# The eighth expert's vector loaded by DMA for every chunk, and the first chunk's state products in two groups

## Chip, cores and metric

One core of one Trainium2 chip (trn2) runs the whole kernel. The metric is device microseconds (us) of one execution; the median of three executions is compared. The profile is one further execution.

## What is computed

Three layers in a row. A linear attention with a decaying state (4 batches, 8 heads, 768 positions, head size 64), a two-layer network (512 to 2048 to 512) with a learned slope for negative values, and a mixture of 8 experts in which each of the 3072 tokens goes to the expert whose embedding has the largest cosine with it:

```python
state = gamma[None, :, None, None] * state + np.einsum('bhd,bhe->bhde', k[:, :, t], v[:, :, t])
y[:, :, t] = scale * np.einsum('bhd,bhde->bhe', q[:, :, t], state)
...
g = np.maximum(h, 0.0) + alpha * np.minimum(h, 0.0)
...
en = expert_emb / (np.linalg.norm(expert_emb, axis=-1, keepdims=True) + 1e-06)
logits = xn @ en.T / tau
expert_idx = np.argmax(logits, axis=1)
...
h = np.maximum(x[mask] @ w1[e], 0.0)
out[mask] = gate_w[mask, None] * (h @ w2[e])
```

## The kernel before

**Stages.** The 768 positions are cut into six chunks (c = 0 to 5) of 128 positions by 4 batches, 512 tokens each. For each chunk TensorE does the attention (`attention`, heads in four pairs, hp = 0 to 3) and then the network (`mlp`, 16 blocks, f = 0 to 15). In a block TensorE does `hidden(c, f + 1)`, 12 matmuls at L750, and then `down(c, f)`, 12 matmuls at L768. Every product is taken of a high and a low part of the numbers, so VectorE, ScalarE and GpSimd make such parts all the time. After chunk 5 come the experts (L843 to L903), some 350 us.

**A block outside TensorE.** VectorE forms `neg` (L1034) and `g` (L1039) from the result of `hidden`, ScalarE copies the high part `g_hi` (L1533, semaphore gh), GpSimd subtracts for the low part `g_lo` (L1784, semaphore gl; VectorE does it in blocks 0 and 15). `down(c, f)` waits for gh before its first matmul and for gl before its fifth.

**The first chunk** (no state yet) also splits the network's weights, one slab n per block: SP loads slab n (`load_w`, L479) into one of two buffers, ScalarE takes the high part (`split_w`, L1509) in block n - 3 behind `g_hi`, VectorE the low part (L985) in the same block. `load_w(n)` waits until slab n - 2 is split. Between blocks TensorE inserts `to_state(0, hp)` (L678), which makes keys times values into the state product of a pair of heads, in a PSUM bank (6 or 7); semaphore SU counts them. VectorE copies each to the state `St` one block later (L1054, semaphore S).

**SP's queue** is one list of transfers in written order, each with its waits ahead of it, so one that waits holds all behind it. In the first chunk `load_w` for n = 4 to 15 is mixed with the next keys and values:

```python
                if n in (7, 10, 13, 15):
                    u = 2 + (7, 10, 13, 15).index(n)
                    load_k(u // HP, u % HP)
                if n in (7, 10, 13):
                    load_v(1, (7, 10, 13).index(n))
```

`load_k` for u = 2, 3, 4, 5 waits for SU of 1, 2, 3, 4 state products, since these read the buffer that it fills. The `load_v` after n = 7, 10, 13 waits for the same count as the `load_k` ahead of it.

**The router** of chunk c runs in the network of chunk c + 1. VectorE takes the dot product of each token with each expert's normalized vector: 32 instructions `scalar_tensor_tensor` of 128x512 (`dots`, L1098), two in blocks 0 and 8, four in blocks 1 to 7. The vectors of experts 0 to 6 lie in SBUF, the same in all 128 partitions, in `EN`. They are written to DRAM by the first chunk (`en_rows`) and loaded with a broadcast once (`spread_en`, L522), in chunk 1. That of expert 7 lies in PSUM (`EN_ps`, bank 7), put there by one matmul (L817) between the first chunk's network and `attention(1)`. The dots write their product, which nobody reads, to `dot_out`, the two halves of the mask buffer `Am`; the sum goes to `L2`. Squares of the rows are taken by ScalarE.

Of the kernel before, what the change touches and what calls it, by code (L numbers as in the profile page):

```python
# [23 lines left out]
P = 128  # L24
# [49 lines left out]
def build(nc, g, where, qk, kv, w_mlp, alpha, emb, tau, w_exp, consts, pad_rows, en_rows, table, out):  # L74
# [10 lines left out]
    TB = B * P  # L85
# [93 lines left out]
    St = part(HP * B * D).rearrange("p (h b c) -> p h b c", h=HP, b=B)  # L179
    assert at[0] == 13 * TB  # L180
    idle_in = A[:, 11 * TB:11 * TB + P]
    dot_out = [A[:, (9 + i) * TB:(10 + i) * TB] for i in range(2)]
    EN = sb("en_all", (E - 1) * DM, f32)
    v_first = by_batch(EN[:, 0:TB])
    qk_first = [EN[:, (1 + 2 * i) * TB:(3 + 2 * i) * TB] for i in range(2)]
# [113 lines left out]
    RK_last = bank[3][:, 0:B * E].rearrange("p (b e) -> p b e", b=B)  # L299
    CNT_first, CNT_ps = bank[6][:, 64:64 + E], bank[7][:, 64:64 + E]  # L300
    SQ_ps = bank[6][:, :]
    EN_ps = bank[7][:, :]
    EMB_ps = bank[5][:, 192:192 + KC * E].rearrange("p (k e) -> p k e", k=KC)
    TAU_ps = bank[5][:, 256:257]
    XT_ps, EH_ps, HT_ps, EY_ps = bank[6], [bank[4], bank[5]], [bank[0], bank[1]], [bank[2], bank[3]]
# [119 lines left out]
    LO_VECTOR_AT = {11: 0, 12: 1, 13: 2, 14: 3}  # L425
    STAR_AT, TURN_AT = 13, FB - 2

    SU_AT = {1 + 3 * hp: hp for hp in range(HP)}

    block = nc.Block()  # L430
    with block:

        @block.sync
        def _(sp):
# [77 lines left out]
                if n in (7, 10, 13):  # L512
                    load_v(1, (7, 10, 13).index(n))
            sp.wait_ge(s_en, due(s_en, 1))
            sp.dma_start(en_rows[0:E - 1, :], emb_sb[0:E - 1, :]).then_inc(s_en_st, 16)
            sp.wait_ge(s_en_st, due(s_en_st, 16))
            sp.wait_ge(s_SU, due(s_SU, HP))
            sp.wait_ge(s_Y, due(s_Y, HP))
            sp.wait_ge(s_en_last, due(s_en_last, 1))

            def spread_en():
                sp.dma_start(EN[:, :], en_rows[0:E - 1, :].rearrange("e d -> (e d)").partition_broadcast(P))\  # L522
                  .then_inc(s_en_all, 16)
                sp.dma_start(table[PAD:PAD + P, :], pad_rows[0:P, :]).then_inc(s_pad0, 16)

            def chunk(c, following=True, with_k=True):

                load_qk(c, 2)
                load_qk(c, 3)
                load_v(c, 3)  # L530
                if following:
                    load_k(c, 2)
                    load_k(c, 3)
                    load_qk(c + 1, 0)
                    load_v(c + 1, 1)
                    load_qk(c + 1, 1)
                if isinstance(c, int) and c == 1:
                    spread_en()
                if following:
                    if with_k:  # L540
                        load_k(c + 1, 0)
                    load_v(c + 1, 2)
                    if with_k:
                        load_k(c + 1, 1)
                    load_v(c + 1, 0)

            chunk(1)
            for e in range(E):
# [76 lines left out]
        def _(pe):  # L625
# [148 lines left out]
            def mlp(c, router_c=None):  # L774


                hidden(c, 0)
                for f in range(FB):
                    if f + 1 < FB:
                        hidden(c, f + 1)  # L780
                    if f == 0 and not is_last(c) and not (isinstance(c, int) and c == 0):
                        pe.wait_ge(s_S, due(s_S, HP * c + HP))
                    down(c, f)
                    if isinstance(c, int) and c == 0 and f in SU_AT:
                        if SU_AT[f] >= 2:
                            pe.wait_ge(s_S, due(s_S, SU_AT[f] - 1))
                        to_state(0, SU_AT[f], SU0_ps[SU_AT[f] % 2])
                    if f == RANK_AT and router_c is not None:
                        router_rank(router_c)

                    if f == RANK_AT + 4 and router_c is not None:
                        pe.wait_ge(s_rk, due(s_rk, router_c + 1))
                    if is_last(c) and f == TURN_AT:
                        pe.wait_ge(s_lg, due(s_lg, B * E * (NC - 1)))
                        x_transpose(0, 0)
                        x_transpose(0, 1)
# [17 lines left out]
            for kc in range(KC):  # L814
                tr(EMB_ps[:, kc, :], emb_sb[0:E, kc * P:(kc + 1) * P], ident[0:E, 0:E])
            mm(TAU_ps, ones[0:1, :], tau_in[0:1, :], start=True, stop=True).then_inc(s_emb, 1)
            mm(EN_ps, ident[0:E, E - 1:E].broadcast_to([E, P]), emb_sb[0:E, :], start=True, stop=True).then_inc(s_en_last, 1)  # L817
            pe.wait_ge(s_ent, due(s_ent, 1))
            pe.wait_ge(s_S, due(s_S, HP))
            attention(1)  # L820
# [128 lines left out]
            e = e_next  # L949
# [27 lines left out]
        def _(dve):  # L977
# [50 lines left out]
            def mlp(c, router_c=None):  # L1028
                for f in range(FB):
# [19 lines left out]
                    elif isinstance(c, int) and c == 0 and f + AHEAD == FB:  # L1049
                        embeddings()  # L1050
                    if isinstance(c, int) and c == 0 and f - 1 in SU_AT:
                        hp = SU_AT[f - 1]
                        dve.wait_ge(s_SU, due(s_SU, hp + 1))
                        ve.tensor_copy(St[:, hp], SU0_ps[hp % 2]).then_inc(s_S, 1)  # L1054
                    if router_c is not None:
                        router(router_c, f)

# [31 lines left out]
            def dots(c, first, count):  # L1089
                if first == 0:  # L1090
                    dve.wait_ge(s_xeV, due(s_xeV, 2 * c + 2))
                    dve.wait_ge(s_xeA, due(s_xeA, 2 * c + 2))
                    dve.wait_ge(s_en_all, due(s_en_all, 16))
                    dve.wait_ge(s_en_last, due(s_en_last, 1))
                for n in range(first, first + count):
                    j, e = n // E, n % E
                    dve.wait_ge(s_lg, due(s_lg, B * E * c + max(n - 1, 0)))
                    ve.scalar_tensor_tensor(dot_out[n % 2], xrow[j][:, 0:DM], 1.0, EN[:, e * DM:(e + 1) * DM] if e < E - 1 else EN_ps,  # L1098
                                            ALU.mult, ALU.mult, accum_out=L2[:, j, e:e + 1]).then_inc(s_lg, 1)

            def router_norm(c):
# [793 lines left out]
```

## Time and profile before

| | |
|---|---|
| three executions | 954.73, 955.74, 956.39 us; median 955.74 |
| the profiled execution | 953.84 us, of which the span of the profile is 951.9 |
| TensorE busy | 939.7 us, 99% of the span, weight loads beside it 799.3 |
| VectorE busy | 648.6 us, 68% |
| ScalarE, GpSimd busy | 304.7 us, 32%; 246.0 us, 26% |
| granted TensorE clock, mean | 0.997 |

The span is the time from the first to the last instruction of the profiled execution; 1.9 us lie around it. The busy share says little of where the kernel waits: for a change, the stage it touches is read in order of time.

### The profile page before, as it was taken

To read this page: it belongs to the slowest core of one execution; us is meant where nothing else is said; L and a number is where in the kernel's file an instruction comes from. 1 tells how busy PE (TensorE), PEld (TensorE's weight loads), DVE (VectorE), ACT (ScalarE), POOL (GpSimd) and SP (SyncE) were. 2 spreads that over 40 slices of the span, in tenths; PEclk is the share of its full clock that TensorE was granted. 3 is DMA by queue.
4 is the path that set the end of the run, shared out by engine and by line. 5 is a ranking of instruction groups with operands and counts; after the bars stand their busy time and mean duration, and the time that the engine had idled before them with its cause. 6 is when DMAs were issued, how large, how long until landed. Compare 5 with 4: busy or idle time off the path is not lost.

```text
span 951.9 us, 16233 instructions
## 1 busy us (share of the span) xinstructions
PE 939.7 (99%) x5702; PEld 799.3 (84%) x5702; DVE 648.6 (68%) x1150; ACT 304.7 (32%) x419; POOL 246.0 (26%) x192
## 2 busy tenths in 40 slices
PE   8999999999999999999999999999999999999996
PEld 7888888888888888888888888899999998888885
DVE  5555579647974698559865887776755557799641
ACT  4222121112111121112111222235555556678541
POOL 4443114341434133412433122520000001100101
PEclk9999999999999999999999999999999999999998
DMA  8431297023001400140002202179866666899611
GB/s 305 163 130 59 78 392 241 1 89 134 0 0 44 176 0 0 44 150 5 1 20 81 111 1 89 46 285 319 331 230 226 227 226 232 316 360 372 237 42 55
DMA packets 32032, 138.44 MB, mean 145 GB/s; under 512 B 5183, under 2 KB 5567, under 8 KB 23248
## 3 DMA queue, kind: packets, MB, share of 16 engines
q1 hardware_dynamic: 24464, 119.20, 34.4%
q0 software_dynamic: 4336, 12.61, 3.4%
q10 hardware_dynamic: 3168, 5.79, 1.9%
q8 instruction: 39, 0.64, 0.3%
q14 instruction: 25, 0.20, 0.1%
HBM read 124.96 MB, written 28.41 MB: 161 GB/s over the span
## 4 chain that ended last, share of the span: by engine, by line
PE 95%; DVE 2%; DMA 1%; issue 1%; ACT 0%; SPq 0%; POOL 0%; POOLq 0%; ACTq 0%; DVEq 0%
PE bank L750 28%; PE bank L768 27%; PE bank L903 14%; PE bank L865 10%; PE bank L843 6%; PE bank L645 2%; PE bank L689 2%; PE bank L661 2%; PE bank L678 1%; DVE weights_split L1259 1%; PE bank L735 1%; PE bank L880 1%; DMA attention<-in_w_exp 1%; DMA attention<-in_qk 1%; PE bank L714 0%
## 5 line engine op out<-in xcount | busy, mean ns | idle before, releaser
L750 PE MATMUL bank<-activations_split,weights_split 128*128 128x512 f32 x1152 | 277.9, 391 | 0.0
L768 PE MATMUL bank<-weights_split,activations_split 128*128 128x512 f32 x1152 | 276.1, 390 | 0.0
L768 PEld LDWEIGHTS bank<-weights_split,activations_split 128*128 128x128 f32 x1152 | 216.3, 188 | 44.7
L750 PEld LDWEIGHTS bank<-activations_split,weights_split 128*128 128x128 f32 x1152 | 215.2, 188 | 45.7 <-issue 0.9
L1784 POOL TENSOR_TENSOR activations_split<-scratch,activations_split 128x512 fp32r<-128x512 f32 x84 | 116.9, 1392 | 310.4 <-ACT activations_split L1533 303.1
L1533 ACT CAST activations_split<-scratch 128x512 fp32r<-128x512 f32 x96 | 59.8, 623 | 412.0 <-DVE scratch L1039 412.0
L903 PE MATMUL bank<-weights_split,activations_split 128*128 128x512 f32 (+1 forms) x648 | 158.2, 396 | 0.0
L1034 DVE TENSOR_SCALAR scratch<-bank,alpha 128x512 f32<-128x512 f32 x96 | 71.8, 748 | 99.2 <-PE bank L750 98.7
L903 PEld LDWEIGHTS bank<-weights_split,activations_split 128*128 128x128 f32 x648 | 118.7, 188 | 23.0
L1098 DVE SCALAR_TENSOR_TENSOR attention<-rows,en_all 128x512 f32<-128x512 f32 x140 | 135.1, 1006 | 0.6 <-DMA en_all<-en_rows 0.6
L1259 DVE TENSOR_TENSOR weights_split<-attention,weights_split 128x2048 fp32r<-128x2048 f32 (+1 forms) x45 | 102.4, 2289 | 23.9 <-ACT weights_split L1613 23.6
L1842 POOL DMA_INDIRECT out<-scratch,y_token x27 | 31.5, 1167 | 277.3 <-ACT scratch L1646 277.3
L865 PE MATMUL bank<-activations_split,weights_split 128*128 128x256 f32 x768 | 94.8, 284 | 0.0
L865 PEld LDWEIGHTS bank<-activations_split,weights_split 128*128 128x128 f32 x768 | 93.6, 192 | 0.6
L1613 ACT CAST weights_split<-attention 128x2048 fp32r<-128x2048 f32 (+1 forms) x45 | 85.5, 1910 | 8.5 <-DMA attention<-in_w_exp 7.0
L1039 DVE SCALAR_TENSOR_TENSOR scratch<-bank,scratch 128x512 f32<-128x512 f32 x96 | 66.4, 692 | 3.3
L843 PE MATMUL bank<-weights_split,activations_split 128*128 x264 | 62.5, 391 | 1.2 <-DVE activations_split L1245 1.0
L843 PEld LDWEIGHTS bank<-weights_split,activations_split 128*128 128x128 f32 x264 | 49.3, 188 | 12.0 <-issue 2.0
L1274 DVE SCALAR_TENSOR_TENSOR activations_split<-bank,activations_split 128x512 fp32r<-128x512 f32 x32 | 22.0, 688 | 37.5 <-ACT activations_split L1660 37.3
L1259 DVE TENSOR_TENSOR weights_split<-en_all,weights_split 128x2048 fp32r<-128x2048 f32 (+1 forms) x15 | 34.4, 2291 | 4.6 <-ACT weights_split L1613 4.6
L1806 POOL DMA_INDIRECT expert_rows<-rows,slot_i x24 | 28.9, 1206 | 30.1 <-DVE slot_i L1198 25.0
L1660 ACT ACTIVATE activations_split<-bank 128x512 fp32r<-128x512 f32 x32 | 19.1, 598 | 49.9 <-PE bank L865 49.9
(243 smaller groups left out, 715.4 us busy)
## 6 DMA issues: line engine op xcount, KB each, us to landing
attention<-in_w_exp SPq DMA_DIRECT2D x48, 1024.0 KB, 6.2
en_all<-in_w_exp SPq DMA_DIRECT2D x16, 1024.0 KB, 7.1
attention<-in_kv SPq DMA_DIRECT2D x43, 256.0 KB, 4.1
expert_rows<-in_pad_rows SPq DMA_DIRECT2D x8, 1285.0 KB, 24.0
rows<-in_w_mlp SPq DMA_DIRECT2D x14, 512.0 KB, 3.5
attention<-in_qk SPq DMA_DIRECT2D x12, 512.0 KB, 5.3
rows<-expert_rows ACTq DMA_DIRECT2D x22, 257.0 KB, 3.3
scratch<-in_qk SPq DMA_DIRECT2D x10, 512.0 KB, 3.9
```

Of the source, the lines that this page charges most:

```text
L750: last = mm(H_ps[f % 2][:, :], win(a, kc, f), x[:, kc, :], start=(k == 0), stop=(k == 3 * KC - 1))
L768: last = mm(bank[j][:, :], x[f % 2][:, j * P:(j + 1) * P], wout(a, f), start=(f == 0 and a == 0 and part_ == "hi"), stop=(f == FB - 1 and ...
L843: last = mm(EH_ps[half][:, :], x[tt % 2][:, kc * P:(kc + 1) * P], W[:, bass.ds(slot * HALF + w1_at(kc, a) + half * 512, 512)], start=(k == ...
L865: last = mm(EH_ps[g % 2][:, j * 2 * P:(j + 1) * 2 * P], W[:, slot + w1_at(kc, a) + fc * P:slot + w1_at(kc, a) + (fc + 1) * P], ex_two[:, b ...
L903: last = mm(EY_ps[tt % 2][:, :], own, W[:, bass.ds(slot * HALF + w2_at(fc, a), DM)], start=(k == 0), stop=(k == 3 * FC - 1))
L1034: ve.tensor_scalar(neg, H_ps[f % 2][:, :], 0.0, alpha_sb[:, f:f + 1], ALU.min, ALU.mult)\
L1039: ve.scalar_tensor_tensor(g_sb[f % 2], H_ps[f % 2][:, :], 0.0, neg, ALU.max, ALU.add)\
L1098: ve.scalar_tensor_tensor(dot_out[n % 2], xrow[j][:, 0:DM], 1.0, EN[:, e * DM:(e + 1) * DM] if e < E - 1 else EN_ps, ALU.mult, ALU.mult, a ...
L1259: ve.tensor_tensor(W[:, bass.ds(at_ + CH, CH)], raw[m], W[:, bass.ds(at_, CH)].bitcast(f32), ALU.subtract).then_inc(s_lo[m // HC], 1)
L1533: se.copy(g_hi[f % 2], g_sb[f % 2]).then_inc(s_gh, 1)
L1613: se.copy(W[:, bass.ds((run % 2) * HALF + raw_at(m), CH)], raw[m]).then_inc(s_hi[m // HC], 1)
L1784: gp.tensor_tensor(g_lo[f % 2], g_sb[f % 2], g_hi[f % 2].bitcast(f32), ALU.subtract)\
```

## The change

1. State products of the first chunk: before, `to_state(0, hp)` stood behind blocks 1, 4, 7 and 10, one in each. Now pairs 0 and 1 stand behind block 4 and pairs 2 and 3 behind block 10. The copies to `St` follow in blocks 5 and 11, two in each.
2. The eighth expert's vector is no longer spread by TensorE into PSUM bank 7. All eight rows go to `en_rows`, and for each chunk 1 to 5 SP loads the eighth with a broadcast (128 partitions by 2 KB) into `en_last`, the second half of `Am`, which attention overwrites each time. The load stands last in the chunk's list and waits for the chunk's last values product (Y). The dots of each chunk wait for it (semaphore en_last, 16 for each load).
3. `dot_out` is now the first half of `Am` and, for every odd dot, PSUM bank 7.
4. SP waits for the embedding's transposes and tau (emb) where it waited for the removed matmul.

```diff
-    dot_out = [A[:, (9 + i) * TB:(10 + i) * TB] for i in range(2)]
+    en_last = A[:, 10 * TB:10 * TB + DM]
...
-    EN_ps = bank[7][:, :]
+    dot_out = [A[:, 9 * TB:10 * TB], bank[7][:, :]]
...
-    SU_AT = {1 + 3 * hp: hp for hp in range(HP)}
+    SU_AT = {4: (0, 1), 10: (2, 3)}
...
-            sp.dma_start(en_rows[0:E - 1, :], emb_sb[0:E - 1, :]).then_inc(s_en_st, 16)
+            sp.dma_start(en_rows[0:E, :], emb_sb[0:E, :]).then_inc(s_en_st, 16)
...
-            sp.wait_ge(s_en_last, due(s_en_last, 1))
+            sp.wait_ge(s_emb, due(s_emb, 1))
...
+            def load_en_last(c):
+                sp.wait_ge(s_Y, due(s_Y, HP * (c + 1)))
+                settle(c)
+                sp.dma_start(en_last, en_rows[E - 1:E, :].rearrange("e d -> (e d)").partition_broadcast(P))\
+                  .then_inc(s_en_last, 16)
...
                     load_v(c + 1, 0)
+                load_en_last(c)
...
-                        if SU_AT[f] >= 2:
-                            pe.wait_ge(s_S, due(s_S, SU_AT[f] - 1))
-                        to_state(0, SU_AT[f], SU0_ps[SU_AT[f] % 2])
+                        for hp in SU_AT[f]:
+                            if hp >= 2:
+                                pe.wait_ge(s_S, due(s_S, hp - 1))
+                            to_state(0, hp, SU0_ps[hp % 2])
...
-            mm(EN_ps, ident[0:E, E - 1:E].broadcast_to([E, P]), emb_sb[0:E, :], start=True, stop=True).then_inc(s_en_last, 1)
...
-                    dve.wait_ge(s_en_last, due(s_en_last, 1))
+                    dve.wait_ge(s_en_last, due(s_en_last, 16 * (c + 1)))
...
-                    ve.scalar_tensor_tensor(dot_out[n % 2], xrow[j][:, 0:DM], 1.0, EN[:, e * DM:(e + 1) * DM] if e < E - 1 else EN_ps,
+                    ve.scalar_tensor_tensor(dot_out[n % 2], xrow[j][:, 0:DM], 1.0, EN[:, e * DM:(e + 1) * DM] if e < E - 1 else en_last,
```

TensorE's instructions in the first chunk, before, from the end of `down(0, 1)` on (L678 is `to_state`; in brackets the semaphores waited for):

```order
L768 MATMUL bank<-weights_split,activations_split 128x512 [waits gl]
L768 MATMUL bank<-weights_split,activations_split 128x512 x7
L678 MATMUL bank<-attention 64x64 [waits vs_first,k_ld0]
L678 MATMUL bank<-attention 64x64 x7
L750 MATMUL bank<-activations_split,weights_split 128x512 [waits g,wlo,whi]
```

And those of the changed kernel from the end of `down(0, 4)` on (its lines are 8 higher here, L686 is `to_state`):

```order
L776 MATMUL bank<-weights_split,activations_split 128x512 [waits gl]
L776 MATMUL bank<-weights_split,activations_split 128x512 x7
L686 MATMUL bank<-attention 64x64 [waits vs_first,k_ld0]
L686 MATMUL bank<-attention 64x64 x7
L686 MATMUL bank<-attention 64x64 [waits vs_first,k_ld1]
L686 MATMUL bank<-attention 64x64 x7
L758 MATMUL bank<-activations_split,weights_split 128x512 [waits g,wlo,whi]
```

The first state product has moved from behind block 1 to behind block 4, and the second follows it at once.

SP's queue in the first chunk, the same in both kernels (L479 is `load_w`: the first row n = 4, the second n = 5 to 7, then `load_k` and `load_v`, then n = 8 to 10):

```order
L479 DMA rows<-in_w_mlp 128x1024 [waits wlo_pool,whi]
L479 DMA rows<-in_w_mlp 128x1024 [waits wlo,whi] x3
L470 DMA attention<-in_kv 128x512 [waits SU]
L462 DMA attention<-in_kv 128x512 [waits SU,Y]
L479 DMA rows<-in_w_mlp 128x1024 [waits wlo,whi] x3
```

No row of it moved; what has moved is the work that SU counts.

SP's queue at the end of chunk 1, before (L549 fills DRAM with padding rows, 8 transfers):

```order
L470 DMA attention<-in_kv 128x512 [waits SU]
L462 DMA attention<-in_kv 128x512 [waits SU,Y]
L470 DMA attention<-in_kv 128x512 [waits SU]
L462 DMA attention<-in_kv 128x512 [waits SU,Y]
L549 DMA expert_rows<-in_pad_rows 32x10280 x8
```

and in the changed kernel:

```order
L471 DMA attention<-in_kv 128x512 [waits SU]
L463 DMA attention<-in_kv 128x512 [waits SU,Y]
L471 DMA attention<-in_kv 128x512 [waits SU]
L463 DMA attention<-in_kv 128x512 [waits SU,Y]
L530 DMA attention<-en_rows 128x512 [waits Y]
L557 DMA expert_rows<-in_pad_rows 32x10280 x8
```

The new load has come in between the last values load and the padding.

## Rows read from the trace of the kernel before

**Rows 1.** The page: shares of the chain that ended last, by engine.

```profile
PE 95%; DVE 2%; DMA 1%; issue 1%; ACT 0%; SPq 0%; POOL 0%; POOLq 0%; ACTq 0%; DVEq 0%
```

**Rows 2.** The chain of waits in the first chunk: start us, us, what.

```profile
48.28 0.61 PE bank L678 x16
48.89 2.95 PE bank L750 x12
...
57.28 2.72 PE bank L768 x12
```

**Rows 3.** SP's queue in the first chunk: start us, us, issue.

```profile
33.83 0.33 SPq L479 DMA_DIRECT2D rows<-in_w_mlp  x1
34.21 0.43 SPq L470 DMA_DIRECT2D attention<-in_kv  x1
34.73 0.38 SPq L462 DMA_DIRECT2D attention<-in_kv  x1
```

**Rows 4.** Landing times from issue, issues of 39 to 40 and of 34.5 to 35 us.

```profile
rows<-in_w_mlp SPq DMA_DIRECT2D x1, 512.0 KB, 3.2
...
attention<-in_kv SPq DMA_DIRECT2D x2, 256.0 KB, 3.9
```

**Rows 5.** ScalarE, VectorE and GpSimd around block 5, in order of time.

```profile
47.63 1.04 ACT L1509 CAST weights_split<-rows 128x1024 fp32r<-128x1024 f32 x1
...
48.71 1.46 DVE L985 TENSOR_TENSOR weights_split<-rows,weights_split 128x1024 fp32r<-128x1024 f32 x1 [1.64 <-ACT weights_split L1509]
50.09 0.41 DVE L1054 COPY attention<-bank 128x256 f32<-128x256 f32 x1
51.88 0.75 DVE L1034 TENSOR_SCALAR scratch<-bank,alpha 128x512 f32<-128x512 f32 x1 [1.37 <-PE bank L750]
...
54.09 1.29 POOL L1784 TENSOR_TENSOR activations_split<-scratch,activations_split 128x512 fp32r<-128x512 f32 x1 [3.02 <-ACT activations_split L1533]
```

**Rows 6.** The chain from the first network's end into attention of chunk 1.

```profile
108.47 0.97 PE bank L817 x2
...
114.81 0.47 PE bank L678 x16
...
134.10 2.72 PE bank L768 x12
```

**Rows 7.** VectorE behind the first network, and its first dot.

```profile
108.62 0.16 DVE L1229 RECIPROCAL tau<-bank 128x1 f32<-128x1 f32 x1
...
129.39 0.69 DVE L1098 SCALAR_TENSOR_TENSOR attention<-rows,en_all 128x512 f32<-128x512 f32 x1 [0.55 <-DMA en_all<-en_rows]
```

**Rows 8.** SP's queue at the end of attention of chunk 1, and one landing (122.8 to 123.2).

```profile
123.02 0.33 SPq L462 DMA_DIRECT2D attention<-in_kv  x1
...
attention<-in_kv SPq DMA_DIRECT2D x1, 256.0 KB, 9.3
```

**Rows 9.** GpSimd in block 1 of chunk 1.

```profile
132.83 1.64 POOL L1784 TENSOR_TENSOR activations_split<-scratch,activations_split 128x512 fp32r<-128x512 f32 x1 [13.12 <-ACT activations_split L1533]
```

**Rows 10.** The dots by form: count, ns min/median/max.

```profile
L1098 DVE SCALAR_TENSOR_TENSOR attention<-rows,en_all x140: 679/686/1785, 129.4 to 571.2; 128x512 f32<-128x512 f32 x140
L1098 DVE SCALAR_TENSOR_TENSOR attention<-rows,bank x20: 679/684/685, 137.5 to 571.8; 128x512 f32<-128x512 f32 x20
```

**Rows 11.** Blocks 1 to 7 of chunk 1, from `neg` to `neg` (columns as in rows 14).

```profile
130.62:167.07 36.45, 36.45 (x163) 30.20 (x162) 36.21 (x71) 6.23 (x13) 15.24 (x10) 1.00 0.83 290
```

**Rows 12.** VectorE: a product of two SBUF inputs written to PSUM, first chunk.

```profile
93.03 0.68 DVE L1203 CUSTOM_DVE_ANT_0 bank<-scratch 8x512 f32<-8x512 f32 x1
```

**Rows 13.** Chunk 2: SP's last load, its landing, and VectorE's first dot.

```profile
224.48 0.93 SPq L462 DMA_DIRECT2D attention<-in_kv  x1
...
attention<-in_kv SPq DMA_DIRECT2D x1, 256.0 KB, 4.2
...
229.92 0.69 DVE L1098 SCALAR_TENSOR_TENSOR attention<-rows,en_all 128x512 f32<-128x512 f32 x1
```

**Rows 14.** The end by windows: us, PE, PEld, DVE, ACT, POOL busy, granted clock, DMA.

```profile
945.00:952.00 7.00, 0.00 (x0) 0.00 (x0) 0.00 (x0) 0.00 (x0) 0.98 (x1) 0.65 0.08 29
```

More of the change, by code:

```diff
@@ L181, in build @@
     idle_in = A[:, 11 * TB:11 * TB + P]
-    dot_out = [A[:, (9 + i) * TB:(10 + i) * TB] for i in range(2)]
+    en_last = A[:, 10 * TB:10 * TB + DM]
+    assert DM <= TB
     EN = sb("en_all", (E - 1) * DM, f32)
@@ L1051, in mlp @@
                     if isinstance(c, int) and c == 0 and f - 1 in SU_AT:
-                        hp = SU_AT[f - 1]
-                        dve.wait_ge(s_SU, due(s_SU, hp + 1))
-                        ve.tensor_copy(St[:, hp], SU0_ps[hp % 2]).then_inc(s_S, 1)
+                        for hp in SU_AT[f - 1]:
+                            dve.wait_ge(s_SU, due(s_SU, hp + 1))
+                            ve.tensor_copy(St[:, hp], SU0_ps[hp % 2]).then_inc(s_S, 1)
                     if router_c is not None:
```

## The prediction

> **What bounds the kernel now.** I read the page first: the chain that ended last runs 95% through TensorE [rows 1], so time is won or lost only where TensorE works less or waits. Then the chain of waits in order of time, for the places that the change touches: in the first chunk it is 2.72 us pieces of 12 matmuls without a gap, `hidden` and `down` in turn, with 0.61 us of state product and a first piece of 2.95 behind it [rows 2]. Last I read the other engines and SP's queue at those places, for how much later each could be before TensorE stands. VectorE's 68% says nothing of that. The sum is made against the profiled execution (953.84 us, span 951.9), which lies 1.9 us below the median of the three runs, 955.74; I add the same difference to both. A difference under 0.2%, 1.9 us, can't be told from no change here.
>
> **What it saves.** An insertion costs TensorE 0.61 us, and the piece behind it is 0.23 longer (2.95 against 2.72): 0.84 [rows 2]. A state product that follows another small matmul group costs 0.47 [rows 6]. So four insertions are 4 x 0.84 = 3.36, two double ones 2 x (0.84 + 0.47) = 2.62: **-0.7 us**. The matmul L817 stands on the chain for 0.97 us [rows 6], but attention behind it waits for VectorE's reciprocal as well, which ends at 108.62 + 0.16 = 108.78 [rows 7]. Attention begins at 108.47 + 0.97 = 109.44; it could at about 108.9: **-0.5 us**, with bounds 0 and 0.97. SP's wait for emb ends earlier than that for the matmul, so nothing is lost there.
>
> **What the moved state products hold up.** SP issues slab 7 at 33.83, then `load_k` at 34.21 and `load_v` at 34.73, whose waits for SU were then long met [rows 3]. Now the first state product ends behind block 4. TensorE is there 0.84 earlier than before, as block 1 has no insertion: 48.28 - 0.84 = 47.44, and the product ends at 48.05. Until then SP stands, and slab 8 is behind in its list. It goes out at 48.05 + (34.73 - 34.21) + 0.52 = 49.1. Slab 7, keys and values landed within 34.73 + 3.9 - 33.83 = 4.8 us of the first issue [rows 3, 4]; the same bytes with the slab last give 48.05 + 4.8 = 52.8, and a slab alone would take 3.2 [rows 4], 52.3. I take 52.7.
>
> ScalarE began to split slab 8 at 47.63 without a wait for it; VectorE followed 1.08 later, had its next instruction 1.38 behind that, and copied a state in 0.41 [rows 5]. Now: ScalarE 52.7, VectorE 53.8, two copies from 55.2, `neg` of block 6 at 56.0. GpSimd's low part ended 54.09 + 1.29 - 51.88 = 3.50 us behind the start of `neg` [rows 5]: 59.5. TensorE, undisturbed, begins `down(0, 6)` at 57.28 - 0.84 + 0.47 = 56.91 and needs the low part four matmuls later (4 x 2.72 / 12 = 0.9), at 57.8. **It stands 1.7 us.** That is not caught up, as its own work is the bound. VectorE has 1.37 us idle in a block [rows 5] and catches up in the next ones; slab 9 goes out right behind slab 8 and is in time.
>
> Behind block 10 it is the same with pairs 2 and 3, slab 13, `load_k(1, 0)` and slab 14, split in block 11: again **+1.7 us**. The sum so far is +2.2.
>
> **What the eighth vector's load does.** In chunk 1 VectorE's first dot already waits, 0.55 us, for the big broadcast, and starts at 129.39 [rows 7]. The new load is issued later: behind the last values load, at 123.02 + 0.33, some 123.4, on a queue that is full. That values load took 9.3 us, to 132.3 [rows 8], where another took 4.2 in chunk 2 [rows 13]. 256 KB more behind it are, at the rate of slab 7 with keys and values (1 MB in 4.8 us with the way there and back), at most 1.2; a slab of 512 KB lands in 3.2 and 256 KB beside it in 3.9 [rows 4], 0.7 later. I take 0.7. So it lands at 133.0, and VectorE's two dots of block 0, with everything behind them, are 3.6 us late. GpSimd's low part of block 1 ended at 132.83 + 1.64 = 134.47 [rows 9]; now 138.1. TensorE needs it at 134.10 + 0.91 = 135.0 [rows 6]. **+3.1 us.** Bounds: below, the load lands with its own 4.2 us, at 127.6, and costs nothing; above, with the 1.2, +3.6.
>
> In chunks 2 to 5 I cost it at nothing: in chunk 2 the last values load lands at 224.48 + 4.2 = 228.7, the new one at some 229.4, the first dot starts at 229.92 [rows 13]. The cover is VectorE's way through `hidden`, `neg` and `g` of block 0, and it is thin, 0.5 us. Without it, a late landing would cost its lateness less what TensorE's low part has to spare in block 1.
>
> **The eighth dot.** Its vector now comes from SBUF. The dots with two SBUF inputs take 679 ns to 1785, those with one in PSUM 679 to 685 [rows 10]: the long ones lie beside GpSimd's instructions. The eighth dot is the second of its block and starts just ahead of GpSimd's low part, which then waits about 0.34 us (1.64 against 1.29 [rows 5, 9]) and holds up the third dot by as much, so VectorE loses 0.33 us in each of four blocks of a chunk. It has some room for that: blocks 1 to 7 of chunk 1 take it 36.45 us without idle time [rows 11], 5.21 each, where TensorE's block is 2 x 2.72 = 5.44. The Trainium skill (SBUF — State Buffer, "Who interferes with whom") has this as a rule: a VectorE instruction with two SBUF inputs contends with a GpSimd one that reads SBUF, and one with at most one doesn't. By that rule, the row agrees. Writing half of the products to PSUM I take as free: such a product took 0.68 us [rows 12]; it had 8 partitions, so a dot could be 0.06 more, as `neg`'s 0.75 is against a dot's 0.69 [rows 5, 7]. In chunk 1, whose VectorE is already late, these may add 0 to 0.7 us; I take +0.1.
>
> **Sum**: -0.7 - 0.5 + 1.7 + 1.7 + 3.1 + 0.1 = +5.4 us. 953.84 becomes 959.2, the median 961.1, 0.56% more.
>
> **Rivals.**
> *The small load is not held by the queue's backlog* (9%). If the eighth vector's 256 KB pass the padding and the loads ahead, no wait of 3.1 arises; it decides at a landing of 129.4 plus 0.5, 129.9, that is 6.5 us after issue instead of 9.6. With slab 8 landing alone, in 3.2 us, each of the two stands is 1.3: -1.2 + 2.6 = +1.4, 957.1, not slower by what can be measured. For it speaks that 4.2 us is what such a load takes in chunk 2 [rows 13]; against it that the one just ahead took 9.3 [rows 8]. The Trainium skill (DMA: Bandwidth & Descriptors, "Queues, rings and completion order") says that a later transfer may complete before an earlier one of the same queue. No row here shows one that passed another.
> *The stands for slabs 8 and 14 don't arise* (8%): if VectorE and GpSimd had more to spare than I read, or the loads landed 1.7 us sooner. -1.2 + 3.2 = +2.0: 957.7. Against it, no load of a slab is under 3.2 us [rows 4].
> *VectorE becomes the bound of the routed blocks* (7%). If each eighth dot takes 1.785 instead of 0.69 [rows 10], four of them in a chunk add 4.4 us, where 5.44 - 5.21 = 0.23 us of each of 8 blocks and, I estimate, 1 us at the start are free, 2.8: 1.6 a chunk, 8 over five, and 969. It decides where an eighth dot costs 0.7 us more. Against it, the second dot of a block is the one that runs undisturbed.
> *The clock falls in a stand* (4%). At the end the granted clock falls to 0.65 on average over 7 us without matmuls [rows 14]. I expect 2.3 us at most in one piece here. If it fell to the lower level of 1.2 GHz for one block, that block would take 5.44 us more: 966.5.
> My forecast has the rest, 72%.
>
> **Numbers.** The forecast's own range comes from its terms: 3.1 may be 2.4 to 3.6, each 1.7 between 1.2 and 2.0, the dots 0 to 0.7, the savings 0.7 to 1.7: +3.1 to +6.9, 958.8 to 962.6. The two rivals below are at 957.1 and 957.7, those above at 966.5 and more. With the upper two (11%) and a little at the lower end left out, the range is 957.2 to 964.0. Slower by over 0.2% (above 957.65): the forecast, both upper rivals, half of the second, some 0.86; within 0.2%: 0.12; faster: 0.02.
>
> **What would show it.** In the changed kernel's trace: SP's `load_k` and `load_v` behind slab 7 at 48 us rather than 34, and slab 8 at 49; TensorE idle before `down(0, 6)` and `down(0, 12)`, 1.7 us each; the first dot of chunk 1 waiting for the load from `en_rows`, 3.6 us later; TensorE idle before `down(1, 1)`, 3.1; state products in pairs, 1.1 us together; no L817. I am wrong if the eighth vector lands before 130 us, if TensorE has no gap in block 6, or if gaps appear in all routed chunks.

## The result, and the profile after

| | before | changed |
|---|---|---|
| executions, median | 955.31 us (4, 954.73 to 956.39) | **968.71 us** (4, 965.70 to 971.66) |
| ratio | | **1.0141** (95%: 1.0126 to 1.0155) |
| the same again, in a later comparison | 955.67 us (7) | 968.22 us (4), 1.0138 (1.0122 to 1.0155) |
| profiled execution, span | 953.84, 951.9 | 971.66, 969.6; the later one 966.37, 964.4 |

Slower by 13 us where 5.4 were forecast. The page of the changed kernel, busy times and then the shares of the chain (before [rows 1]):

```profile
PE 945.0 (97%) x5700; PEld 802.9 (83%) x5700; DVE 652.4 (67%) x1150; ACT 305.4 (31%) x419; POOL 251.1 (26%) x192
...
PE 92%; DMA 4%; DVE 2%; ACT 1%; issue 1%; SPq 0%; POOL 0%; POOLq 0%; DVEq 0%; ACTq 0%
```

The reader is to see that the chain has lost 3% of TensorE and gained 3% of DMA, and that TensorE's busy time is 5 us up (945.0 against 939.7) though the page counts two matmuls fewer (5700 against 5702): part of the loss is idle time, part is matmuls that took longer. Where, TensorE's rows say; in brackets the idle time ahead and what ended it. I call such an idle time a stand:

```profile
47.43 1.15 PE L686 MATMUL bank<-attention 128*64 128x64 f32 x32
...
59.48 4.67 PE L776 MATMUL bank<-weights_split,activations_split 128*128 128x512 f32 x12 [2.52 <-ACT activations_split L1541]
...
98.46 5.49 PE L776 MATMUL bank<-weights_split,activations_split 128*128 128x512 f32 x12 [3.08 <-ACT activations_split L1541]
...
148.31 4.82 PE L776 MATMUL bank<-weights_split,activations_split 128*128 128x512 f32 x12 [4.92 <-ACT activations_split L1541]
```

The three late ones are `down(0, 6)`, `down(0, 12)` and `down(1, 1)`, the places of the forecast, and the only stands in the network. The idle time is 10.5 us; the twelve matmuls behind it take 4.7 to 5.5 us where they took 2.88 by the same view before:

```profile
57.12 2.88 PE L768 MATMUL bank<-weights_split,activations_split 128*128 128x512 f32 x12
```

The granted clock (last column but two) in them and in stretches around:

```profile
59.50:64.00 4.50, 4.50 (x13) 3.34 (x14) 2.82 (x3) 1.58 (x3) 3.52 (x3) 0.62 0.54 181
...
98.40:104.00 5.60, 5.54 (x13) 4.38 (x14) 4.51 (x7) 1.57 (x3) 2.32 (x2) 0.50 0.01 1
...
148.30:153.00 4.70, 4.69 (x13) 3.60 (x14) 4.67 (x9) 1.04 (x3) 1.62 (x1) 0.59 0.96 315
```

The clock had fallen to its lower level, 0.5 of 2.4 GHz, for most or all of each. For over 35 us ahead of each stand, but for the stand before, TensorE had run with no gap over 0.4 us, and in the stand it was idle.

The chain through the first stand, read from below:

```profile
48.15 0.33 SPq L471
...
48.57 0.38 SPq L463
...
49.05 5.35 DMA rows<-in_w_mlp
...
54.42 1.06 ACT weights_split L1517
...
56.64 0.75 DVE attention L1062 x2
57.39 0.67 DVE scratch L1042
...
58.81 0.63 ACT activations_split L1541
59.48 4.67 PE bank L776 x12
```

`down` waits for `g_hi` on ScalarE, that for `neg` and `g` on VectorE, these for VectorE's part of the split and its two state copies, and all of it for slab 8, which SP issued at 49.05 behind `load_k` and `load_v`; those stood until the state product of 47.43 was done (before, they went out at 34.21 and 34.73 [rows 3]). The same chain leads into the second stand from slab 14, and into the third from the eighth vector's load:

```profile
87.47 0.85 SPq L480 DMA_DIRECT2D rows<-in_w_mlp  x2
...
93.39 1.05 ACT L1517 CAST weights_split<-rows 128x1024 fp32r<-128x1024 f32 x1 [8.03 <-DMA rows<-in_w_mlp]
...
132.67 0.43 SPq L530 DMA_DIRECT2D attention<-en_rows  x1
...
144.90 0.69 DVE L1106 SCALAR_TENSOR_TENSOR attention<-rows,en_all 128x512 f32<-128x512 f32 x1 [6.78 <-DMA attention<-en_rows]
```

**How far TensorE is behind.** I read the starts of the same matmuls, each kernel's minus those of the kernel before. Where a row names a `down`, it is the start of the first matmul behind it. L743 are the first transposes for the experts, in block 15 of chunk 5 (L735 in the kernel before). The changed kernel has two profiled executions, the second being e11_again below:

| place | forecast | first | second |
|---|---|---|---|
| `down(0, 6)` | +1.3 | +4.1 | +1.9 |
| `down(0, 12)` | +2.7 | +9.6 | +5.95 |
| start of attention(1) | +2.2 | +9.4 | +5.42 |
| `down(1, 1)` | +5.4 | +16.3 | +10.5 |
| L743 | +5.4 | +16.3 | +10.6 |
| end of the span | +5.4 | +17.7 | +12.5 |

From chunk 1 to chunk 5 nothing is added. The two executions differ by 5.8 us at the third stand, as much as their times do (971.66 and 966.37). The changed kernel's four executions spread over 6 us where those of the one before spread over 2 (over 3 in the later comparison); that the others differ for the same reason is not shown, since only these two were profiled. The last 1.4 and 1.9 us arise in the experts. From L743 to the end it is 340.8 us before, 342.1 and 342.7 here, and between 340.3 and 343.2 in the profiled executions of the experiments, whatever they changed: that part belongs to the execution, not to the change. So the start of L743 is the sharper measure, and I give it beside the times of some experiments.

A profiled execution also reaches `down(0, 1)`, which lies ahead of everything that the change and the experiments touch on TensorE, at a time of its own: 28.23 us before, 28.30 and 28.59 in the two above, 28.1 to 28.8 in the experiments, and 30.14 in e12_busy_all. Where a few tenths matter I therefore also give the shift from `down(0, 1)` to the start of attention(1), with that difference taken off.

### The profile page after: what moved, and what is told of

Read it like the earlier page. It is cut to its first block, busy times and chain, and to the rows that moved or that the text cites. A ratio compares the mean times of both kernels' runs of the same rounds, so it can differ in the third digit from the quotient of the medians.

```text
span 969.6 us, 16236 instructions
## 1 busy us (share of the span) xinstructions
PE 945.0 (97%) x5700; PEld 802.9 (83%) x5700; DVE 652.4 (67%) x1150; ACT 305.4 (31%) x419; POOL 251.1 (26%) x192
## 4 chain that ended last, share of the span: by engine, by line
PE 92%; DMA 4%; DVE 2%; ACT 1%; issue 1%; SPq 0%; POOL 0%; POOLq 0%; DVEq 0%; ACTq 0%
PE bank L776 27%; PE bank L758 25%; PE bank L911 14%; PE bank L873 10%; PE bank L851 6%; PE bank L653 2%; PE bank L697 2%; PE bank L669 2%; DMA attention<-en_rows 1%; PE bank L743 1%; DMA rows<-in_w_mlp 1%; PE bank L686 1%; PE bank L888 1%; DMA attention<-in_w_exp 1%; DVE weights_split L1267 1%; DMA attention<-in_qk 1%
## 5 line engine op out<-in xcount | busy, mean ns | idle before, releaser
L776 PE MATMUL bank<-weights_split,activations_split 128*128 128x512 f32 x1152 | 282.4, 396 | 10.5 <-ACT activations_split L1541 10.5
L1792 POOL TENSOR_TENSOR activations_split<-scratch,activations_split 128x512 fp32r<-128x512 f32 x84 | 123.7, 1472 | 315.0 <-ACT activations_split L1541 315.0
L1106 DVE SCALAR_TENSOR_TENSOR attention<-rows,en_all 128x512 f32<-128x512 f32 x80 | 92.7, 1158 | 6.8 <-DMA attention<-en_rows 6.8
L1106 DVE SCALAR_TENSOR_TENSOR bank<-rows,en_all 128x512 f32<-128x512 f32 x60 | 53.5, 892 | 0.0
L993 DVE TENSOR_TENSOR weights_split<-rows,weights_split 128x1024 fp32r<-128x1024 f32 x13 | 18.4, 1412 | 35.8 <-ACT weights_split L1517 35.8
```

The costliest lines, as they stand in the source:

```text
L776: last = mm(bank[j][:, :], x[f % 2][:, j * P:(j + 1) * P], wout(a, f), start=(f == 0 and a == 0 and part_ == "hi"), stop=(f == FB - 1 and ...
L1792: gp.tensor_tensor(g_lo[f % 2], g_sb[f % 2], g_hi[f % 2].bitcast(f32), ALU.subtract)\
```

## Experiments

Ratios are to the kernel before in the same comparison; "at L743" is how much later (+) or sooner (-) the profiled execution came there than that of the kernel before.

**Each half alone.** e1_states is the kernel before with the first of these edits and nothing else (and `to_state` in a loop over the pairs), e2_vector the changed kernel with the second, so that only the vector is changed:

```diff
-    SU_AT = {1 + 3 * hp: hp for hp in range(HP)}
+    SU_AT = {4: (0, 1), 10: (2, 3)}
...
-    SU_AT = {4: (0, 1), 10: (2, 3)}
+    SU_AT = {1: (0,), 4: (1,), 7: (2,), 10: (3,)}
```

> Only the state products in pairs (behind blocks 4 and 10); the eighth vector stays in PSUM bank 7 as before. Late slabs with a clock fall behind each stand: TensorE idle before down(0, 6) and down(0, 12), 2.5 and 3 us, the matmuls behind each at the lower clock, together +7 to +10 us. Late slabs alone, without a part of the clock: +4 to +5.5. If the loss of the changed kernel came from the vector's load and the dots: -0.7.

> Only the eighth vector's load for every chunk; the state products one behind each of blocks 1, 4, 7, 10 as before. One late landing in chunk 1: a single stand of TensorE before down(1, 1), 4 to 5 us, with the clock fall +4.5 to +7 in all, and none in chunks 2 to 5. If the dots' contention with GpSimd or their writing to PSUM were the cost: gaps of TensorE in every routed chunk, and +1 us or more in each.

e1_states: 963.27 us (4), 1.0088 (1.0071 to 1.0105), at L743 +7.4. e2_vector: 960.71 (4), 1.0057 (1.0040 to 1.0074), +5.9. The sum, 1.45%, agrees with the 1.41% of the whole: these intervals show no interaction of the halves. e1 has the two stands in the first chunk and none in chunk 1; TensorE's rows and two windows:

```profile
59.84 4.51 PE L768 MATMUL bank<-weights_split,activations_split 128*128 128x512 f32 x12 [3.04 <-ACT activations_split L1534]
...
98.27 1.19 PE L768 MATMUL bank<-weights_split,activations_split 128*128 128x512 f32 x4 [2.67 <-ACT activations_split L1534]
99.65 2.12 PE L768 MATMUL bank<-weights_split,activations_split 128*128 128x512 f32 x8 [0.18 <-POOL activations_split L1785]
...
59.84:62.40 2.56, 2.56 (x6) 2.10 (x7) 1.63 (x2) 0.90 (x1) 2.53 (x2) 0.50 0.64 242
98.20:101.80 3.60, 3.34 (x13) 2.47 (x14) 2.56 (x3) 0.98 (x2) 1.30 (x1) 1.00 0.01 2
```

After an idle time of 3.04 us the clock was at its lower level; after one of 2.67 it stayed at the upper, and the matmuls took their usual time. e2 has one stand, in chunk 1, and none in chunks 2 to 5:

```profile
137.06 5.49 PE L776 MATMUL bank<-weights_split,activations_split 128*128 128x512 f32 x12 [3.51 <-ACT activations_split L1541]
```

**The slab stands: is it the order of SP's queue?** In e3_order the state products are moved, and the keys and values loads are put behind slabs 9, 10 and 15. The first of them still wait, until 48.11, but slabs 8 and 9 have gone out ahead of them, and slab 10 goes out at 49.41 (before at 50.24):

```diff
-                if n in (7, 10, 13, 15):
-                    u = 2 + (7, 10, 13, 15).index(n)
+                for u in {9: (2,), 10: (3,), 15: (4, 5)}.get(n, ()):
...
-                if n in (7, 10, 13):
-                    load_v(1, (7, 10, 13).index(n))
+                    if u < 5:
+                        load_v(1, u - 2)
```

> State products in pairs as in e1_states, but the keys and values that wait for them stand behind slab 9, slab 10 and slab 15 in SP's list instead of behind slabs 7, 10, 13 and 15. If the list's order is what holds the slabs up: no stand, no clock fall, -0.7 us against before. If the double product itself delays VectorE or TensorE: at least +2 us remains.

954.64 us (10), 0.9993 (0.9984 to 1.0003), at L743 -0.9, and no stand. `down(0, 6)` at its place, with 2.88:

```profile
56.76 2.88 PE L767 MATMUL bank<-weights_split,activations_split 128*128 128x512 f32 x12
```

So all of e1's 8 us come from slabs 8 and 14 lying behind the transfers that wait for SU, and none from the paired insertions themselves. The forecast saving of 0.7 us is not told from zero by the times; in the profiled execution it is there, 0.75 us from `down(0, 1)` to attention(1).

e6_early kept SP's list and moved the pairs to blocks 1 and 7 (`SU_AT = {1: (0, 1), 7: (2, 3)}`), so that no state product comes later than before.

> State products in pairs behind blocks 1 and 7 (pairs 0 and 1, then 2 and 3), never later than before; all else as before. If lateness in SP's list was the whole cost of the pairs: no stand, and the saving of two insertions, -0.7 us (954.6 for 955.3). If a double product delays the next block by VectorE's two copies: +0.5 us or more.

955.23 us (12), 1.000 (0.999 to 1.001), at L743 -0.8, no stand, and again 0.75 us saved from `down(0, 1)` to attention(1). Two remedies of one cause, with one result.

**Why the slab landed later than 3.7 us from its issue.** In e9_alone (the state products alone moved) slab 9 is not issued before slab 8 has landed, nor 15 before 14:

```diff
+                if n in (8, 14):
+                    sp.wait_ge(s_wld[wbuf(n)], due(s_wld[wbuf(n)], 16 * wload(n)))
```

> e1_states, but slab 9 is not issued before slab 8 has landed, nor slab 15 before slab 14. If slab 9, issued 0.4 us behind slab 8, shares the queue with it and so made it land after 5.9 us instead of my 3.7: slab 8 lands in 3.3 to 4.0 us, each stand is 1.5 to 2 us shorter, +4 to +5 us against before instead of +8. If only what is ahead of a transfer delays it: 5.9 us as in e1_states and the same time.

960.75 us (7), 1.0045 (1.0029 to 1.0061): nearly half of e1's loss is gone. Landing of slab 8 from issue in e1 and in e9, and TensorE's rows in e9:

```profile
rows<-in_w_mlp SPq DMA_DIRECT2D x1, 512.0 KB, 5.9
```

```profile
rows<-in_w_mlp SPq DMA_DIRECT2D x1, 512.0 KB, 4.5
...
58.77 1.21 PE L770 MATMUL bank<-weights_split,activations_split 128*128 128x512 f32 x4 [1.71 <-ACT activations_split L1536]
...
94.89 1.19 PE L770 MATMUL bank<-weights_split,activations_split 128*128 128x512 f32 x4 [1.40 <-ACT activations_split L1536]
96.26 3.68 PE L770 MATMUL bank<-weights_split,activations_split 128*128 128x512 f32 x8 [0.18 <-POOL activations_split L1787]
...
96.20:99.80 3.60, 3.54 (x9) 2.78 (x10) 3.50 (x7) 0.62 (x1) 0.40 (x2) 0.53 0.00 0
```

The stands are half as long, though the landings, 4.5 us and 4.2 for slab 14, are not quite the 3.3 to 4.0 that I had expected. So the slab issued right behind, one that nobody needed yet, delayed the one that TensorE waited for. The rest, 4.5 against the 3.7 that I took, is with keys and values ahead. The last row shows the clock falling after a stand of only 1.40 us.

Nor need the neighbour be a slab. Slab 10 had keys and values 0.4 us behind it in the kernel before, and ahead and behind in e3, and landed in

```profile
rows<-in_w_mlp SPq DMA_DIRECT2D x1, 512.0 KB, 5.1
```

```profile
rows<-in_w_mlp SPq DMA_DIRECT2D x1, 512.0 KB, 5.4
```

So the trace of the kernel before held a row of over 5 us. It is not a rule, either: with the same neighbours behind them slabs 7 and 13 landed there in 3.3 and 3.8.

**The third stand: the load's place or the padding?** Both have the vector alone. e5_front issues chunk 1's load right behind the big broadcast, ahead of one padding transfer (257 KB) and four keys and values loads; e7_pads leaves it and holds the eight padding transfers behind it until it has landed:

```diff
+                    load_en_last(c)      # e5_front, chunk 1, behind spread_en
+                    load_pad()
...
+            sp.wait_ge(s_en_last, due(s_en_last, 16))      # e7_pads, ahead of the padding
```

> e2_vector with chunk 1's load of the eighth vector right behind the big broadcast in SP's list, ahead of the padding row and the four key and value loads of chunk 2 (these then wait for the attention's end too). If the 1.3 MB ahead of it in the queue make it late: it lands some 4 us earlier against attention's end than in e2_vector, TensorE stands 0 to 2 us, +0 to +2 us in all. If a broadcast of one 2 KB row is slow in itself or the padding behind holds it: still 10 us or more from issue to landing and a stand of over 3 us.

> e2_vector with the eight padding transfers (1285 KB each) held until the eighth vector has landed. If the padding issued behind it slows its landing: 9.6 us or less from issue to landing instead of 12, the stand shorter by 2 us. If only what is ahead counts: still 12 us, the same time as e2_vector within 1 us.

e5_front: 955.38 us (10), 1.000 (0.999 to 1.001), at L743 -0.5, no stand. e7_pads: 959.91 (4), 1.0044 (1.0029 to 1.0059), the stand still there. The first dot of chunk 1 in e2, e5 and e7:

```profile
133.65 0.69 DVE L1106 SCALAR_TENSOR_TENSOR attention<-rows,en_all 128x512 f32<-128x512 f32 x1 [5.37 <-DMA attention<-en_rows]
```

```profile
129.00 0.69 DVE L1111 SCALAR_TENSOR_TENSOR attention<-rows,en_all 128x512 f32<-128x512 f32 x1 [0.63 <-DMA attention<-en_rows]
```

```profile
134.21 0.69 DVE L1107 SCALAR_TENSOR_TENSOR attention<-rows,en_all 128x512 f32<-128x512 f32 x1 [5.00 <-DMA attention<-en_rows]
```

The load lands 10.6 us after issue in e2, 10.2 in e7 and 6.2 in e5, and the issues lie close together (122.85, 123.77 and 122.57): it is what lies ahead in the queue that delays it. What the padding behind adds is small and not settled: in e7 the big broadcast itself took 12.1 us against 10.6 in e2, and the load landed 3.8 us behind it against 4.6. At the front the first dot starts 4.6 us sooner, and the change costs nothing.

**What is the fallen clock worth?** e4_busy is e1 with `hidden(0, 7)` and `hidden(0, 13)` done twice, so that TensorE has work in the two slab stands; e12_busy_all is the same edit in the changed kernel, beside that kernel once more (e11_again).

```diff
+                if isinstance(c, int) and c == 0 and f in (7, 13):
+                    k = 0
+                    for kc in range(KC):
+                        for a, x in ((0, x_hi), (0, x_lo), (1, x_hi)):
+                            last = mm(H_ps[f % 2][:, :], win(a, kc, f), x[:, kc, :],
+                                      start=(k == 0), stop=(k == 3 * KC - 1))
+                            k += 1
```

> e1_states with hidden(0, 7) and hidden(0, 13) each done twice (24 matmuls for 12, the same result), so that TensorE works where it stood. If the clock falls because TensorE stands: granted clock 1.00 through both places, down(0, 6) and down(0, 12) begin about when they did in e1_states and take 2.9 us, and the kernel is 3 to 5 us faster than e1_states though it does more. If the clock has no part: equal to e1_states or up to 1 us slower.

> The changed kernel once more, for its spread on one chip beside e12_busy_all: 966 to 972, 968.7 in the middle, if the clock falls by chance in some stands and not in others; within 2 us if it always falls.

> The changed kernel with hidden(0, 7) and hidden(0, 13) done twice, as in e4_busy, so that TensorE hardly stands in the first chunk. If the fallen clock behind the two stands costs 1 to 2 us each: 2 to 4 us faster than e11_again, the third stand as it was. If it costs nothing: equal, or up to 1 us slower.

e4_busy: 962.49 us (4), 1.0068 (1.0046 to 1.0090), 0.8 under e1. e11_again: 968.22 (4, 966.37 to 969.91), the spread that was expected if the clock falls in some stands and not in others. e12_busy_all: 968.35 (4), 1.0132 (1.0115 to 1.0149). I had foretold larger gains, and these intervals overlap: as a price of the clock the pair decides nothing. The traces say why. The repeats did what they should, idle time 0.32 and 0.56 us and the clock at 1.00 in both places of e4:

```profile
60.44 1.20 PE L775 MATMUL bank<-weights_split,activations_split 128*128 128x512 f32 x4 [0.32 <-ACT activations_split L1541]
...
98.42 1.19 PE L775 MATMUL bank<-weights_split,activations_split 128*128 128x512 f32 x4 [0.56 <-ACT activations_split L1541]
```

but they are 2 x 2.72 = 5.4 us of work, and e11, the execution to compare with, had less to win than the first one. TensorE in e11, with two windows:

```profile
58.40 1.20 PE L776 MATMUL bank<-weights_split,activations_split 128*128 128x512 f32 x4 [1.14 <-ACT activations_split L1541]
59.76 2.12 PE L776 MATMUL bank<-weights_split,activations_split 128*128 128x512 f32 x8 [0.16 <-POOL activations_split L1792]
...
95.89 4.39 PE L776 MATMUL bank<-weights_split,activations_split 128*128 128x512 f32 x12 [2.79 <-ACT activations_split L1541]
...
142.39 1.38 PE L776 MATMUL bank<-weights_split,activations_split 128*128 128x512 f32 x4 [2.84 <-ACT activations_split L1541]
144.09 3.29 PE L776 MATMUL bank<-weights_split,activations_split 128*128 128x512 f32 x8 [0.32 <-POOL activations_split L1792]
...
58.40:61.80 3.40, 3.24 (x13) 2.37 (x14) 2.43 (x3) 0.90 (x1) 3.37 (x2) 1.00 0.41 155
95.89:100.11 4.22, 4.22 (x12) 3.42 (x13) 3.26 (x4) 1.30 (x2) 1.28 (x1) 0.65 0.01 2
```

Slab 8 landed in 4.0 us here, not 5.3; the first stand was 1.14 us, without a fall of the clock. In its first two stands together 1.14 + 2.79 us were idle and 0.9 lost to the clock, 4.8: less than the repeats cost. In the first execution it was 2.52 + 3.08 and 3.5, 9.1. Counted from `down(0, 1)` to the start of attention(1) the first execution is 9.3 us behind the kernel before, the second 5.1, and e12 lies between, 6.2: the same edit would have won 3 us against the one and lost 1 against the other. Besides, e12's profiled execution had come to `down(0, 1)` 1.9 us late, ahead of any edit.

The clock can be priced in a second way. Mean granted clock over all the timed executions of a comparison, and the time not granted, (1 - clock) x span, each time a mean:

| kernel | executions | not granted, us | above before |
|---|---|---|---|
| before (beside e11, e12) | 7 | 2.2 | |
| changed, both comparisons | 8 | 6.9 | 4.7 |
| e1_states | 4 | 4.3 | 2.3 |
| e2_vector | 4 | 4.8 | 2.8 |
| e4_busy | 4 | 2.2 | 0.2 |
| e12_busy_all | 4 | 4.8 | 2.6 |
| e3_order | 10 | 2.1 | 0.1 |

This counts idle time at a low clock too, so I take it as an upper bound for the mean. From the rows: between the start of a late `down` and the next `hidden` there lie 4.50, 5.29 and 4.65 us in the first execution and 3.31, 4.22 and 4.82 in the second, where 2.72 are undisturbed and 3.31 is one with the low part's wait at full clock (0.6). That leaves 4.5 us for the clock in the one, 4.9 with the `hidden` behind the second stand, whose twelve matmuls took 0.34 longer than usual, and 2.4 in the other. I estimate the clock's part at 2.4 to 4.7 of the 13 us; the lower figure is that of one execution.

**The whole change with both remedies**: e8_both has e3's order and e5's front place, e10_early_front e6's blocks and e5's place.

> The whole change with both lists put right: keys and values that wait for state products behind slabs 9, 10 and 15, and chunk 1's load of the eighth vector right behind the big broadcast. If the order of SP's list is all that cost time: no stand, and the savings of the change remain, two insertions and the matmul, -1.2 us against before (a ratio of 0.9987), near what can be measured. If the per-chunk load, the dots' contention or PSUM writes cost something too: at or above the time of before.

> The same with the state products in pairs behind blocks 1 and 7 in place of the other order of the keys' loads: again no stand and -1.2 us if lateness was all; a difference from e8_both would say that where the pairs stand matters in itself.

e8_both: 954.47 us (12), 0.9990 (0.9978 to 1.0002), at L743 -0.1. e10_early_front: 955.20 (12), 0.9993 (0.9983 to 1.0004), -0.9. No stand in either. From `down(0, 1)` to attention(1) both save 1.3 us, as the forecast's 0.7 + 0.5 say. That is all the change is worth with its three waits gone, and no version beats the kernel before by an amount that its time can show.

## Why the prediction was wrong, and where it was right

The direction (slower) and the places held; the time did not, 961.1 against 968.7. Two terms failed: the landing of the slabs, taken too short, and the fallen clock, put at nothing in the sum.

**Right.** *SP's queue*: `load_k` and `load_v` at 48.15 and 48.57, forecast 48; slab 8 at 49.05, forecast 49.1. *The three places*: idle time before `down(0, 6)`, `down(0, 12)` and `down(1, 1)` and nowhere else in the network, each with the chain of causes that was given; e3 and e6 show it for the first two by taking the cause away, e5 for the third. *The savings*: 0.7 for the insertions and 0.5 for L817. From `down(0, 1)` to attention(1), e3 and e6 save 0.75 us, e2, e5 and e7 save 0.55, and e8 and e10 save 1.29; in the table of shifts L817's part is the step from +5.95 to +5.42. *Chunks 2 to 5 cost nothing*: the shift is +16.3 at 153 us and +16.3 at L743. *The eighth dot*: it costs VectorE some 0.33 us in its block and does not make it the bound. The third dot of such a block took 1.44 us before and takes 1.77 now, and GpSimd's low part beside it 1.63 instead of 1.29, as forecast. The eighth dot and the one behind it, before and in e11:

```profile
137.55 0.69 DVE L1098 SCALAR_TENSOR_TENSOR attention<-rows,bank 128x512 f32<-128x512 f32 x1
...
138.16 1.44 DVE L1098 SCALAR_TENSOR_TENSOR attention<-rows,en_all 128x512 f32<-128x512 f32 x1
```

```profile
147.12 0.69 DVE L1106 SCALAR_TENSOR_TENSOR bank<-rows,attention 128x512 f32<-128x512 f32 x1
...
147.73 1.77 DVE L1106 SCALAR_TENSOR_TENSOR attention<-rows,en_all 128x512 f32<-128x512 f32 x1
```

**Wrong: the landing of the slabs, "I take 52.7".** That was 3.7 us from issue, bounded by 3.2, from a slab alone, and 3.8, from three transfers with nothing behind them. In the changed kernel SP has fallen behind, so slab 9 goes out 0.4 us after slab 8, and the two share the queue. Measured: slab 8 landed in 5.3 us and in 4.0, slab 14 in 5.9 and 5.6, against 4.5 and 4.2 without the neighbour (e9). The 5.1 us of slab 10 in the kernel before would have warned of it. I wrote that slab 9 "goes out right behind slab 8 and is in time"; I asked what that did for slab 9 and not what it did to slab 8. Where the landing was 4.0, the first place cost 1.14 us and 0.6 for the low part, 1.7, as forecast. So this part of the sum was right and its input was not.

**Wrong: the fallen clock, put at nothing in the sum, and at 4% as a rival.** It held in three stands of three in one execution and in two of three in the other. Its price was too high, though: a whole block at half speed, 5.44 us, where a fall cost 0.9 to 2.3, and the `hidden` behind the late `down` was at most 0.34 longer than usual. The sentence behind the 4% was "I expect 2.3 us at most in one piece"; the pieces were 1.1 to 4.9 us. But the size is not all: the clock stayed up after 2.67 us in e1 and fell after 1.40 us in e9. The row from which I argued [rows 14] shows that it falls in 7 us without matmuls, and bounds nothing below. No row of before had TensorE idle for 1 to 3 us in the network, so there was no ground for a chance near zero; and the clock belonged to the forecast as a term that each stand may carry, not as a rival that excludes it.

**The third stand, +3.1**: right in e11, where the load landed in 9.9 us (taken: 9.6) and the stand was 2.84 + 0.32 = 3.16. In the first execution it landed in 12.0, above my upper bound, and the stand was 4.9. The clock came on top in both. In e2, the vector alone, the time rose 5.5 us, of which up to 2.8 is clock by the table: the rest meets the forecast's -0.5 + 3.1 + 0.1 = 2.7.

**The rival "the small load is not held by the queue's backlog"** is refuted by 12.0, 10.6, 10.2 and 9.9 us behind the backlog against 6.2 in front of it. The Trainium skill (DMA: Bandwidth & Descriptors, "Queues, rings and completion order") allows a later transfer to complete first; no landing that I read here shows one that did.

**The sum, mended.** In the second execution: idle 1.14 + 2.79 + 2.84, three low-part waits of 0.6, and 2.4 for the clock are 11.0; less 1.2 saved, 9.8, where the shift from `down(0, 1)` to L743 is 10.2. In the first: 10.5 + 1.8 + 4.9 - 1.2 = 16.0, where it is 16.3.

**A slip in the forecast's own range.** Its terms give 3.6 + 2.0 + 2.0 + 0.7 - 0.7 = +7.6 at the upper end, not +6.9: the 0.7 of the dots was left out. And its "no load of a slab is under 3.2 us" is not quite so, since two took 3.1 in the kernel before. Neither changes the outcome.

**Open.** Why slab 8 landed in 5.3 us in one execution of the kernel and in 4.0 in another, and the eighth vector in 12.0 and 9.9, with the same transfers around them; and what decides whether the clock falls in a stand of 1 to 3 us. The share of the clock is an estimate (2.4 to 4.7 us) and not a value: the experiments on it cost about as much work as they save.

## What to carry to other kernels

Work that a semaphore counts can't be moved without a look at every transfer queued behind the first wait for that count: here the state products cost nothing where they went (e3, e6), and 8 us by what stood behind two waits in one in-order list. A transfer that becomes late may be followed at once by the next (slab 9 here) and be delayed by it, so its landing is to be taken from rows with neighbours ahead and behind, with their spread, and not from the quiet ones. When a bound engine that ran without a gap gets stands of microseconds, price each with and without the fallen clock; and put the load that is needed first at the front of the list.

## What the hardware showed that I had not expected

- The granted clock was at its lower level, for all or part of the twelve matmuls, behind stands of 1.40, 2.52, 2.79, 2.84, 3.04, 3.06 (e12), 3.08, 3.14 (e7), 3.51 and 4.92 us, and at the upper behind 1.14, 1.71 and 2.67. The length of the stand alone doesn't sort them. In some the first four matmuls still ran at or near full speed and the next eight didn't (e9's second place, 1.19 and 3.68 us; e11's third, 1.38 and 3.29).
- A slab of 512 KB with keys and values just ahead landed in 5.3 to 6.1 us with another slab issued 0.4 us behind it (nine landings in five executions, and one of 4.0), and in 4.5 and 4.2 with none behind. With nothing ahead, and keys and values behind, it was 3.3, 3.8 and 5.1 in the kernel before; with nothing around it 3.2 [rows 4].
- The read of a dot's sum takes longer when the product goes to PSUM, 0.135 us against 0.080, and the dot is 693 ns against 683. Not all of the 10 ns is PSUM: odd dots of chunk 1 in the kernel before, with the product in SBUF, took 686 to 690. Rows of such instructions of the changed kernel: count, ns min/median/max:

```profile
L1106 DVE SCALAR_TENSOR_TENSOR attention<-rows,en_all x80: 679/683/1783, 144.9 to 587.5; 128x512 f32<-128x512 f32 x80
L1106 DVE DVE_READ_ACCUMULATOR attention<-rows,en_all x80: 75/80/84, 145.5 to 588.2; 128x1 f32 x80
L1106 DVE SCALAR_TENSOR_TENSOR bank<-rows,en_all x60: 687/693/1779, 145.5 to 585.0; 128x512 f32<-128x512 f32 x60
L1106 DVE DVE_READ_ACCUMULATOR bank<-rows,en_all x60: 132/135/143, 146.1 to 585.6; 128x1 f32 x60
```

So writing the product to PSUM was not quite free, as I took it; VectorE had the room.
